# Attention scores as stacked fp32r products: q scaled and both operands split on GpSimd, three slots, no bias instruction, transposes between the score tiles

## What is computed

```python
# q, k, v: (4, 8, 576, 64); tau = 0.02
scores = scale * np.matmul(q, k.transpose(0, 1, 3, 2))        # scale = 1/8
thresh = np.max(scores, axis=-1, keepdims=True) - tau
scores = np.where(scores >= thresh, scores, -1000000000.0)
scores = scores - np.max(scores, axis=-1, keepdims=True)
attn = np.exp(scores)
attn = attn / (np.sum(attn, axis=-1, keepdims=True) + 1e-09)
x = np.matmul(attn, v)                                         # (4, 8, 576, 64)
h = x.reshape(2304, 512) @ w_in                                # first layer, w_in (512, 1024); ...
```

## Time and profile before

| | before |
|---|---|
| median of 3 runs | 962.96 us (960.71 to 964.64) |
| the profiled execution's own time | 962.48 us |
| its span | 960.7 us |
| TensorE, VectorE, ScalarE, GpSimd busy | 95%, 82%, 52%, 44% |

### The profile page before, as it was taken

How to read it: one execution, slowest core, us unless ns; L and a number is a source line. 1 busy time by engine, 2 the same in 40 slices (tenths; PEclk the granted TensorE clock), 3 DMA queues, 4 the chain that set the end, 5 groups by cost and what they waited for, 6 DMA issues and landing times.

```text
span 960.7 us, 14851 instructions
## 1 busy us (share of the span) xinstructions
PE 915.0 (95%) x5168; PEld 735.4 (77%) x5168; DVE 783.1 (82%) x1517; ACT 502.8 (52%) x936; POOL 423.1 (44%) x439
## 2 busy tenths in 40 slices
PE   4899999999999899999999889999999999999997
PEld 2555565565566579889889878899999999999996
DVE  5889889889885493763754299999999999999997
ACT  2667666667775363442434265545545545455453
POOL 1333333333454281412412065655555556555553
PEclk9999999999999899999999999999999999999999
DMA  9224224124210010000000260000000000000000
GB/s 244 74 48 95 53 50 98 47 55 99 70 45 23 1 45 1 1 1 1 1 1 12 64 208 25 1 34 1 33 1 1 33 1 1 33 0 0 33 0 33
DMA packets 27874, 37.55 MB, mean 39 GB/s; under 512 B 2336, under 2 KB 15648, under 8 KB 27808
## 3 DMA queue, kind: packets, MB, share of 16 engines
q1 hardware_dynamic: 27520, 36.41, 13.7%
q10 hardware_dynamic: 288, 0.30, 0.1%
HBM read 31.98 MB, written 4.72 MB: 38 GB/s over the span
## 4 chain that ended last, share of the span: by engine, by line
DVE 52%; PE 38%; issue 6%; ACT 3%; DMA 1%; POOL 0%; SPq 0%; DVEq 0%
DVE g L823 12%; PE y_ps L995 10%; PE s_ps L905 8%; DVE g_hi L827 7%; PE o_ps L944 7%; DVE g L813 7%; DVE g_lo L829 6%; PE t_ps L917 5%; PE h_ps L884 5%; DVE g L816 5%; DVE top L677 3%; DVE kept L696 2%; DVE x_lo L672 2%; ACT expd L481 2%; DVE solu L780 1%
## 5 line engine op out<-in xcount | busy, mean ns | idle before, releaser
L423 POOL TENSOR_TENSOR w_lo<-w_raw,w_hi 128x512 fp32r<-128x512 f32 x96 | 131.7, 1372 | 161.3 <-ACT w_hi L599 159.2
L390 POOL TENSOR_SCALAR kept<-kept,inv 128x576 f32<-128x576 f32 x144 | 105.9, 753 | 185.6 <-DVE inv L712 185.6
L481 ACT ACTIVATE expd<-s_ps,bias 128x576 f32<-128x576 f32 x144 | 107.6, 747 | 95.7 <-DVE bias L682 95.7
L905 PE MATMUL s_ps<-k_sb,q_sb 64*128 64x288 f32 x640 | 111.8, 456 | 23.7 <-DVE kept L696 14.3
L971 PE MATMUL m_ps<-y_hi,w_lo 128*128 128x384 f32 x384 | 130.9, 341 | 0.0
L971 PE MATMUL m_ps<-y_lo,w_hi 128*128 128x384 f32 x384 | 129.8, 338 | 0.0
L677 DVE TENSOR_REDUCE top<-s_ps 128x1 f32<-128x576 f32 x144 | 108.5, 753 | 24.8 <-PE s_ps L905 24.2
L971 PE MATMUL m_ps<-y_hi,w_hi 128*128 128x384 f32 x384 | 128.5, 335 | 0.0
L615 ACT ACTIVATE l<-u 128x384 f32<-128x384 f32 x96 | 50.4, 525 | 145.8 <-POOL u L431 145.8
L431 POOL TENSOR_TENSOR u<-z,consts 128x384 f32<-128x384 f32 x96 | 105.9, 1103 | 41.8 <-ACT z L608 41.7
L1052 PE MATMUL f_ps<-w_hi,g_hi 128*128 128x512 f32 x288 | 115.4, 401 | 9.2 <-DVE g_lo L829 9.2
(11 more groups left out here) (82 smaller groups left out, 1841.0 us busy)
## 6 DMA issues: line engine op xcount, KB each, us to landing
q_sb<-q_t SPq DMA_DIRECT2D x32, 288.0 KB, 5.2
k_sb<-k_t SPq DMA_DIRECT2D x30, 144.0 KB, 5.6
v_sb<-v_main SPq DMA_DIRECT2D x16, 256.0 KB, 3.3
stage<-w_in SPq DMA_DIRECT2D x16, 256.0 KB, 2.7
w_raw<-w_out SPq DMA_DIRECT2D x8, 512.0 KB, 6.4
out<-o_sb SPq DMA_DIRECT2D x5, 768.0 KB, 3.5
stage<-w_in SPq DMA_DIRECT2D x4, 512.0 KB, 9.1
stage<-w_out SPq DMA_DIRECT2D x4, 512.0 KB, 3.6
```

Source lines behind the costliest of these rows:

```text
L390: nc.gpsimd.tensor_scalar(kept[:, tile % RING, :], kept[:, tile % RING, :], inv[:, group % 2, k:k + 1], 1.0, ALU.mult, ALU.mult).then_inc( ...
L423: nc.gpsimd.tensor_tensor(w4[1][:, n % 2, :], w4_raw[:, n % F2, :], f32(w4[0][:, n % 2, :]), ALU.subtract).then_inc(w4lo_made, 1)
L481: nc.scalar.activation(expd[:, tile % 2, :].rearrange("p (a b) -> p a b", a=2), s_ps[tile % 2][:, :, 0:HALF], ACT.Exp, bias=bias[:, tile % ...
L905: last = nc.tensor.matmul(s_ps[tile % 2][:, a, 0:HALF], q_sb[halves[a], slot, at:at + P], k_sb[halves[a], slot, image, :], start=(n == 0), ...
```

## The change

- q is multiplied by 1/8 ahead of the products; q and k are each split into an fp32r part and the rest, on GpSimd (`scale_q`, `round_q`, `split_q`, `round_k`, `split_k`), between its groups of `kept` tiles. Pair 0 is split by VectorE and ScalarE. Pair 1 is split on GpSimd ahead of the loop.
- SyncE loads q and k raw (147 KB an image) and then copies the parts within SBUF into three slots: q's two parts in both halves of the partitions (`spread_q`, four DMAs of 295 KB), k's first part in the lower half and its rest in the upper (`spread_k`, four of 147 KB): 1.77 MB a pair. ScalarE's queue does so for k of pair 0.
- A score tile is four fp32r products with all 128 rows of contraction (288 columns each), eight in a two-term tile.
- `maximum` gives the negated maximum, which is the exponential's bias: `make_bias` goes; both thresholds follow the second maximum.
- ScalarE does both exponentials of a double ahead of the copies.
- TensorE puts three transposes between the two score tiles; `hidden(1, 1)` moves behind the whole loop. `kept` has six buffers where it had eight; the gain and the later weights are loaded after the last score.

```diff
+SLOTS = 3
-RING = 8
+RING = 6
...
+        def spread_q(engine, pair):
+            source, slot = parts_of(pair)[0], pair % SLOTS
+            for image in range(2):
+                for half in halves:
+                    at = image * (SEQ + LEFT)
+                    engine.dma_start(f32(q_hl[half, slot, :, at:at + SEQ]), f32(source[halves[image], :, :])
+                                     ).then_inc(q_ready[slot], 16)
...
-            load_scores(0)
+            load_q(0)
+            load_q(1)
             sp.dma_start(tau_sb[:, :], tau_d.partition_broadcast(P)).then_inc(tau_in, 16)
-            load_scores(1)
+            sp.wait_ge(q0_split, 1)
+            spread_q(sp, 0)
+            load_q(2)
+            sp.wait_ge(k0_split, 1)
+            load_k(2)
+            sp.wait_ge(q_split, 1)
+            spread_q(sp, 1)
+            sp.wait_ge(k_split, 1)
+            spread_k(sp, 1)
+            for pair in range(4):
                 load_values(pair)
...
+            for pair in range(2, PAIRS):
+                sp.wait_ge(q_split, pair)
+                if pair >= SLOTS:
+                    sp.wait_ge(s_made, scored(pair - SLOTS))
+                spread_q(sp, pair)
+                sp.wait_ge(k_split, pair)
+                spread_k(sp, pair)
...
+                if pair is not None:
+                    if n in (0, 3):
+                        round_k(pair)
+                        split_k(pair)
+                    if n in (1, 4):
+                        scale_q(pair)
+                    if n in (1, 5):
+                        round_q(pair)
+                    if n in (2, 5):
+                        split_q(pair)
...
+                for tile in (2 * v - LAG_T, 2 * v + 1 - LAG_T):
+                    if 0 <= tile < TILES:
+                        transposed(tile)
...
                 if a < TILES:
-                    make_bias(a)
+                    maximum(b)
                     make_thresh(a)
-                    maximum(b)
-                if a < TILES:
-                    make_bias(b)
                     make_thresh(b)
...
+                for a in range(2):
+                    for n, (image, at) in enumerate(terms):
+                        for part in range(2):
+                            last = nc.tensor.matmul(s_ps[tile % 2][:, a, 0:HALF], q_hl[:, slot, part, at:at + P],
+                                                    k_hl[:, slot, image, a * HALF:(a + 1) * HALF],
...
+                old = 2 * v - LAG_T
+                if 2 * v < TILES:
+                    scores(2 * v)
+                if 0 <= old < TILES:
+                    transpose(old, range(0, 3))
+                if 2 * v < TILES:
+                    scores(2 * v + 1)
+                if 0 <= old < TILES:
+                    transpose(old, range(3, KT + 1))
+                    transpose(old + 1, range(0, KT + 1))
...
+            pe.wait_ge(xlo_made, 2)
+            hidden(1, 1)
```

More of the change, by code:

```diff
@@ L115, in build @@
         p_sb = sb("p_sb", [P, KT + 1, PCOLS * P], where=phase)
[L116 to L118 removed]
+        ntop = sb("ntop", [P, 4], where=phase)
         thresh = sb("thresh", [P, 4], where=phase)
@@ L246, in place, with scored, parts_of @@
             g, h, k = n // SIX, n % SIX // GROUP, n % GROUP
-            return 2 * (unit % 2) + h, GROUP * g + k
+            return 2 * unit + h, GROUP * g + k
+        def scored(pair):
+            return UNIT * (pair // 2) + UNIT - (GROUP if pair % 2 == 0 else 0)
+        def parts_of(pair):
+            if pair == 1:
+                return [p_sb[:, n, 0:2 * SEQ].bitcast(FP32R).rearrange("p (a c) -> p a c", a=2) for n in range(2)]
+            return q_parts[:, :, :], k_parts[:, :, :]
         def after_product(i, n):
@@ L387, in _ @@
+            for group in range(GROUPS):
+                unit, n = divmod(group, UNIT // GROUP)
+                if n < 4 and unit + 1 < UNITS:
+                    pair = 2 * (unit + 1) + (n > 0)
+                elif n >= 4 and unit + 2 < UNITS:
+                    pair = 2 * (unit + 2)
+                else:
+                    pair = None
                 pool.wait_ge(inv_made, group + 1)
@@ L453, in _ @@
         def _(act):
-            for a in range(2):
-                act.dma_start(k_sb[halves[a], 0, :, :], k_d[0, :, :, a * HALF:(a + 1) * HALF]).then_inc(k_in[0], 16)
+            for pair in range(2):
+                for image in range(2):
+                    act.dma_start(k_raw[halves[image], pair, :], k_d[pair, :, image, :]).then_inc(k_in[pair], 16)
             nc.scalar.preload_act_table_set("natural_log_exp_and_others")
+            act.wait_ge(k_in[0], 32)
+            nc.scalar.copy(k_parts[:, 0, :], k_raw[:, 0, :]).then_inc(k0_rounded, 1)
+            act.wait_ge(k0_split, 1)
+            spread_k(act, 0)
             def w_high(n):
@@ L889, in scores @@
             def scores(tile):
-                slot, t = place(tile)
+                pair, t = place(tile)
+                slot = pair % SLOTS
                 if tile % UNIT in (0, GROUP):
-                    for loaded in (q_in, k_in):
-                        pe.wait_ge(loaded[slot], 32 * (tile // (2 * UNIT) + 1))
+                    for ready in (q_ready, k_ready):
+                        pe.wait_ge(ready[slot], 64 * (pair // SLOTS + 1))
                 if t < KT:
@@ L902, in scores @@
                 wait(pe, kept_made, tile - 1)
[L903 to L922 removed]
+                for a in range(2):
[3 more added lines that the diff above has]
+                                                    k_hl[:, slot, image, a * HALF:(a + 1) * HALF],
+                                                    start=(n == 0 and part == 0),
+                                                    stop=(n == len(terms) - 1 and part == 1))
@@ new lines, in scores, with transpose @@
+                last.then_inc(s_made, 1)
+            def transpose(tile, blocks):
+                if 0 in blocks:
+                    pe.wait_ge(probs_made, tile + 1)
+                    wait(pe, p_made, tile - 1)
+                    if tile % 2 == 0:
+                        wait(pe, l_made, tile // 2)
+                for k in blocks:
+                    if k < KT:
+                        nc.tensor.matmul(t_ps[tile % 2][:, k * P:(k + 1) * P],
+                                         kept[:, tile % RING, k * P:(k + 1) * P], ident[:, :], is_transpose=True,
+                                         start=(k == 0), stop=(k == KT - 1))
+                    else:
+                        at = (tile % 2) * P
+                        nc.tensor.transpose(l_ps[:, at:at + P], kept[:, tile % RING, SEQ - P:SEQ], ident[:, :]
+                                            ).then_inc(t_made, 1)
```

171 lines of the change are left out of this document (95 added, 76 removed).

## The result

The changed kernel takes **1054.15 us** (median of 4, 1052.22 to 1054.94) where the kernel before takes 963.47 in the same runs (median of 4, 960.71 to 964.64): a ratio of 1.0943, 95% interval 1.0914 to 1.0972. That is slower, on the side that the forecast gave 0.52, but 70 us outside its range. The side is luck for the most part: the forecast had it for the longer start, some 12 us, and most of the 91 us come from something that it had put at nothing.

What follows compares the result with a forecast made beforehand. TensorE and VectorE, within a tenth of each other in a loop of scores, maximum, exponential and keep, were taken to bound the kernel. 962.48 + 1 + 11.8 - 5.2 = 970.1, as a median 970.6 us; range 951 to 984.

Steps and rivals of the forecast that it cites:

- GpSimd and copies in steady state: Attention units: GpSimd's splits and the copies within SBUF fit beside other work, costed at nothing.
- ring and unit: Attention: a double of 3.95 us makes a unit 36.4 us against 36.33; eight units, +1 us.
- start: Before steady attention: loading, splitting and copying the first pairs brings double 2 to 28.7 us; +11.8 us.
- end of attention: Moving `hidden(1, 1)` behind the loop starts the maximum of row tile 1 earlier; -5.2 us.
- GpSimd ... I cost it at nothing: GpSimd in attention: splits plus scaling take 24 of 36 us a unit; no cost, 4 us if uncovered.
- Copies in steady state ... I cost nothing: Attention DMA: two pairs' transfers take 21 of 36 us a unit; no cost.
- a wait ... of transposes for GpSimd would prove the covers thin: Sign within attention units: TensorE's transposes waiting for GpSimd would show its work is not safely hidden; no size given.
- slower yet: Rival: copies at 170 GB/s, or GpSimd's two-input passes taking longer beside VectorE; 985 us or more, chance 0.09.
- The ring: Attention double: maximum, exponential, two copies, `l_ps` copy, transposes, scores, next maximum in turn; 3.94 us, taken as 3.95.
- the first rival: Attention: ScalarE's copy is out of the way, TensorE's own work rules, 33.1 us a unit; 950 us, chance 0.21.
- The rival of fast copies: Copies within SBUF run well above the loads' rate; double 2 at some 22 us, start +6, 965 us; chance 0.17.

Runs made afterwards that it cites:

- version 1: The changed kernel with SyncE's wait on `o_made` and the v loads moved behind the even pair's copies; 976.47 us, ratio 1.0133.
- version 2: version 1 with TensorE waiting for the `l_ps` copy only ahead of the block that writes `l_ps`; 960.43 us, ratio 0.9972.
- version 3: version 1 with ScalarE back at exponential, copy, exponential, copy, TensorE's wait staying early; 964.84 us, ratio 1.0017.
- version 7: version 2 with pair 1's copies issued ahead of pair 2's raw loads; 965.53 us, ratio 1.0031.
- version 8: version 7 with ScalarE's order of the kernel before (exponential, copy, exponential, copy); 963.29 us, ratio 1.0010.
- version 9: version 2 with pair 2's q copies issued ahead of the values of pairs 2 and 3 and the stage loads; 960.58 us, ratio 0.9978.
- version 10: version 9 with pair 1's copies also issued ahead of pair 2's raw loads; 955.86 us, ratio 0.9935.
- version 4: The kernel before with only `hidden(1, 1)` moved behind the attention loop; 957.44 us, ratio 0.9934.
- version 5: The kernel before, fp32 scores kept, with three transposes between score tiles, the early `l_ps` wait and both exponentials first; 991.84 us, ratio 1.0313.

## Why the prediction was wrong

By its own steps, with what each measured:

| term | forecast | measured |
|---|---|---|
| GpSimd and copies in steady state | 0 | +77.7 |
| ring and unit | +1 | +4.3 |
| start | +11.8 | +14.2 |
| end of attention | -5.2 | -4.8 |

The first is the changed kernel less version 1, the second 8 x (36.87 - 36.33), the third double 2 at 30.05 less 15.89, the fourth the way from the last pair of scores to the maximum of row tile 1, 27.88 us against 32.66. They add to 91.4; the medians differ by 90.7 (the first term is taken across two groups of runs, whose own medians of the kernel before differ by 1.0).

**The step that failed** is "GpSimd ... I cost it at nothing" together with "Copies in steady state ... I cost nothing". Both were sums of durations (24 of 36 us, 21 of 36 us), and as sums they hold: version 1 has the same work and, from unit 1 on, no wait of GpSimd for a copy. The cost itself is what failed: the runs showed 77.7 us in the place of nothing, some 13 in each of six units. What I didn't do is walk SyncE's queue in its new order. The odd pair's pass ends with a wait on `o_made`, met only when the unit before has all its values. In the stretch shown, the double at 132.14 us is the sixth of its unit, so the unit began near 112: the wait is met 24 us in. The even pair's copies stand behind it, and GpSimd comes to the rounding that needs them 18 us in. I looked for lateness at the readers of `q_hl` (tile 3, the odd pair) and named no reader of `q_parts`. The statement that "a wait ... of transposes for GpSimd would prove the covers thin" was the right thing to look for, and no rival had its price: the nearest, "slower yet", took the copies to be slow.

**The ring** was right in kind and short by little. Start to start, in the timelines of the changed kernel: maximum to exponential 0.79 (forecast 0.79), exponential 0.64 (0.64), two copies 0.94 (0.93), `l_ps` copy to first transpose 0.54 (0.45), transposes 0.27 (0.37), scores to the next maximum 0.81 (0.76): 3.99 against 3.94. The rows of it, from the timelines of VectorE, ScalarE and TensorE, in order of time:

```profile
126.05 0.76 DVE L791 TENSOR_REDUCE ntop<-s_ps 128x1 f32<-128x576 f32 x1 [0.99 <-PE s_ps L1014]
126.84 0.74 ACT L586 ACTIVATE expd<-s_ps,ntop 128x576 f32<-128x576 f32 x1 [1.07 <-DVE ntop L791]
127.48 1.06 ACT L595 COPY p_sb<-t_ps 128x512 f32<-128x512 f32 x2
128.42 0.40 ACT L608 COPY p_sb<-l_ps 128x256 f32<-128x256 f32 x1
128.96 0.52 PE L1029 MATMUL t_ps<-ident,kept 128*128 128x128 f32 x3
129.23 0.77 PE L1014 MATMUL s_ps<-k_hl,q_hl 128*128 128x288 f32 x4
130.04 0.76 DVE L791 TENSOR_REDUCE ntop<-s_ps 128x1 f32<-128x576 f32 x1 [0.31 <-PE s_ps L1014]
```

The forecast's unit was summed with 3.95; nine times the 0.04 that were short are 0.36 of the 0.47 by which a unit passes 36.4. (In the rival's price a ring of 3.7 gives 952 by the forecast's own sum, and not 954.) Versions 2 and 3 show that this ring was the limit, and the first rival ("the old pair stays the limit") false for the kernel as changed; it holds for version 2, at 34.65 a unit and not 33.1, since a short double takes 3.58 and not 3.15.

**The start** was mis-sized: first scores at 18.5 for 17, tile 3 at 26.85 for 25.4; and the 1 us that the first doubles were to save does not show. From 8 to 16 and from 16 to 24 us the engines moved 220 and 237 GB/s, copies and pair 2's raw loads together, where I took 254 of the loads. The rival of fast copies is false: the page "DMA: Bandwidth & Descriptors" of the Trainium skill (Where 436 GB/s comes from) would allow 435 GB/s; the trace shows 238 from 142 to 146 us, where almost nothing but copies moved, with the engines' share at 0.96. So these copies into half of the partitions filled the engines at about half of that rate. Versions 7 to 10 show that the start also held a smaller stall of the same kind, in unit 0.

**The end** was right, by version 4 alone too.

**What the parts of the change were worth:** the products and the missing bias, in the old order, 0.9 us a unit; the new order of TensorE and ScalarE another 0.75 a unit with the late wait, and with the early one a ring that costs 16 us (29 in the kernel before); the end 5; the price of it all is the start, 14 us (11 in version 10, where double 2 begins at 26.78), which eats most of what the scores win: the best version with fp32r scores (10) is no faster than version 4. What stays open is why version 9's executions differ by 6 us among themselves, and where 2.2 of the 9.7 us between versions 7 and 10 come from.

## What to carry to other kernels

For every wait in a queue, ask when it is met in us from the start of the unit, and then who waits for each thing issued behind it; a sum of busy times and bytes, however far under the period, says nothing on that. Buffers have two kinds of readers: look at who may overwrite the source of a copy as well as at who reads its target. A wait that guards one small buffer belongs right ahead of the instruction that writes it.

## What the runs showed of the hardware

- fp32 score products on two halves of the array (version 5) and fp32r ones on the full array (changed kernel) took the same 0.8 us from their start to the maximum (0.80 and 0.81). Three transposes hold 0.45 us ahead of the first and 0.27 ahead of the second.
- TensorE's granted clock fell to 0.50 (1.2 GHz) in a stall of 10.5 us, and three transposes behind it took 0.90 us where three take 0.52. At the start four score products took 1.33 us where they take 0.79 later, and there the view gives a granted clock of 1.00 (16 to 24 us): its value there does not tell their pace.
- Copies from SBUF to SBUF, 288 and 144 KB each (KB as on the page) into 64 partitions, ran at 238 GB/s with the engines' share at 0.96 (142 to 146 us). At the start, mixed with raw loads, the engines moved 220 and 237 GB/s, where the kernel before moved 254 and 309 with loads alone.
- Four q copies took about 3.8 us to issue on SyncE's queue within the units. At the start, where the two queues issued in overlapping stretches, four took up to 6.0 us on ScalarE's (version 8) and 7.0 on SyncE's (version 7).
